# Three small groups of matmuls of a fused attention and feed-forward kernel, moved into one place of its hand-written order

## The chip, the cores and the metric

The kernel runs on one core of a Trainium2 chip. The metric is the device time of one execution in microseconds; lower is better. Times are given as the median of several runs.

## What is computed

From `reference.py`, cut to what matters. Shapes: q, k, v (8, 8, 576, 64), p (8, 8, 32, 64); all float32.

```python
def sm_attn(qq, kk, vv):
    s = scale * np.matmul(qq, kk.transpose(0, 1, 3, 2))
    s = s - np.max(s, axis=-1, keepdims=True)
    a = np.exp(s)
    a = a / (np.sum(a, axis=-1, keepdims=True) + 1e-09)
    return np.matmul(a, vv)
p_packed = sm_attn(p, k, v)            # 32 packed rows per head
out = sm_attn(q, p_packed, p_packed)   # 576 tokens per head
# out -> x of (4608, 512), then _moe_ref and _moe2_ref:
xn = x / sqrt(mean(x * x) + 1e-06) * rms_g
g = xn @ w_gate                        # 512 x 1536
val = xn @ w_val
x = (g * sigmoid(g) * val) @ w_out     # 1536 x 512
h = x @ w_in                           # 512 x 2048
return (maximum(h, 0) + alpha * minimum(h, 0)) @ w_out2
```

## The kernel before, in words

There are two stages. The first works through the 8 batches, each in two half tiles of 288 tokens (`tile(b, half, at)`); the second stage, a loop over 9 tiles of 512 tokens, isn't touched. The order of each engine's work is written out by hand, engine by engine, and the engines meet at semaphores.

A half tile is a loop over f, the 12 chunks of 128 hidden columns. For each f TensorE computes a gate product (6 large matmuls of 288 columns into PSUM bank 0) and a val product (6 more, bank 1). Each large product is three passes of a high and a low part (`three_passes`, lines 580 to 582). ScalarE takes the silu of the gate (line 964), VectorE multiplies it with val ("mult", line 1213), ScalarE rounds the result to its high part ("h_hi", line 970), VectorE subtracts for the low part ("h_lo", line 1216). From f=2 on TensorE follows with the down product of chunk f-2: 12 large matmuls into the four y banks, 4 to 7. The next gate waits for the silu before it, the next val for the mult before it, since each has only one bank. At the end of a half tile VectorE and ScalarE evict the y banks (lines 1224, 978, 980) and SyncE stores them.

The weights of the gate and val products are not w_gate and w_val. Since the second attention's probabilities times the packed rows come ahead of them, the kernel multiplies the weights by the packed rows first: the six weight products of a batch, `fold0` to `fold5`, each 8 small matmuls of 512 columns on 64x32 tiles of the array (line 712; a float32 matmul has two records in the trace, so 16). They go to banks 2 and 3 and are cast to `m_hi` (ScalarE, line 929) and subtracted to `m_lo` (VectorE, line 1163), two instructions on each engine. fold5 makes chunks 10 and 11.

While batch b is in its tiles, the attention of batch c = b + 1 is prepared between the large matmuls. Tables say at which place which step stands: `PE_PLACES`, `DVE_PLACES`, `ACT_PLACES`, keyed by (half, where, f), with "ready" (ahead of the last three val matmuls), "within" (behind the gate), "after" (behind the val product), "between" (behind the down product). `PE_FIRST` and its like add the late steps of batch 0 in the first tile. The steps that matter here:

- `scores0`, `scores1`: the two halves of p times k, each 8 small matmuls of 288 columns on 64x32 tiles (line 600), in banks 2 and 3 at f=1 and f=2 of half 0. ScalarE copies each half to `a_sb` (line 871).
- `max0`, `max1` at f=2: VectorE's maximum over `a_sb` and a small scaling (lines 1040, 1043). `exp0`, `exp1` behind f=3: ScalarE's exponentials (line 876), which need another activation table than silu, so there is a table load ahead of them and one ahead of silu 4.
- `split(b, 1)`: the high (ScalarE, line 917, at f=1) and low part (VectorE, line 1156, at f=2) of the second half's activations.
- `fold5` of batch c at (1, "between", 11), the end of half 1.

A run of steps on small tiles between large matmuls is called a visit below.

Of the kernel before, what the change touches and what calls it, by code (L numbers as in the profile page):

```python
# [15 lines left out]
PACK = 32  # L16
# [24 lines left out]
PE_PLACES = {  # L41
    (0, "ready", 1): ["scores0_ready"], (0, "after", 1): ["scores0"],
    (0, "ready", 2): ["scores1_ready"], (0, "after", 2): ["scores1"],
    (0, "after", 5): ["turn_a01"], (0, "between", 5): ["turn_a2"], (0, "between", 6): ["packed"],
# [9 lines left out]
}  # L54
# [9 lines left out]
    (1, "between", 8): ["fold3"], (1, "within", 10): ["split0"], (1, "between", 10): ["fold4"],  # L64
    (1, "between", 11): ["fold5"],
}
ACT_PLACES = {
    (0, "between", 1): ["scores0"], (0, "between", 2): ["scores1"], (0, "after", 3): ["exp0", "exp1"],
    (0, "between", 5): ["turn_a0"], (0, "within", 6): ["turn_a2"],
    (0, "within", 8): ["packed"], (0, "after", 11): ["probs"], (0, "between", 11): ["silu"],  # L70
    (1, "between", 1): ["fold0"], (1, "between", 3): ["fold1"], (1, "after", 6): ["rsqrt"], (1, "between", 6): ["fold2"],
    (1, "between", 8): ["fold3"], (1, "between", 9): ["split0"], (1, "between", 10): ["fold4"], (1, "between", 11): ["fold5"],
}
# [8 lines left out]
ACT_FIRST = {  # L82
    (0, "after", 0): ["fold5", "fold4"], (0, "between", 6): ["rsqrt1"], (0, "within", 9): ["split1"],
}
EARLY_BANK, LATE_BANK = 7, 0
# [9 lines left out]
def build(nc, q_t, k_t, v_s, p_t, w1_gv, w1_o, w2, rms_g, alpha, out_t):  # L95
# [3 lines left out]
    with ExitStack() as ctx:  # L99
# [137 lines left out]
        gate_ps, val_ps = psum[:, 0, 0:HALF], psum[:, 1, 0:HALF]  # L237
        scores_ps = psum[:, 2:4, 0:HALF]
        pp_ps, ppt_ps = psum[:, 3, 0:P], psum[:, 2, 0:P]
# [4 lines left out]
        def first(c):  # L244

            return isinstance(c, int) and c == 0
# [27 lines left out]
        def m_bank(c, j):  # L274

            return [4, 6, 4, 2, 6, 4][j] if first(c) else 2

        def scores0_of(g):
# [69 lines left out]
        def tiles_of_a(eng, tile, beside):  # L348

            table, starting = {"PE": (PE_PLACES, PE_FIRST), "DVE": (DVE_PLACES, DVE_FIRST),  # L350
                               "Activation": (ACT_PLACES, ACT_FIRST)}[eng.engine.name]

            def places_of(c, half):
                def at(where, f):
                    if c == 1:
                        for name in starting.get((half, where, f), []):
                            beside(0, name)
                    if c < BATCH:
                        for name in table.get((half, where, f), []):
                            beside(c, name)  # L360
                return at

            for b in range(BATCH):
                for half in range(2):
                    tile(b, half, places_of(b + 1, half))
# [211 lines left out]
        def _(pe):  # L577
# [6 lines left out]
            def scores_ready(c, h):  # L584

                pe.wait_ge(k_in[h], 16 * (c + 1))
                if h == 0:
                    pe.wait_ge(p_in, 16 * (c + 1))
                    if c > 0:
                        pe.wait_ge(m_lo_done, evicted(c))  # L590
                elif c > 0:
                    pe.wait_ge(scores_out, 2 * (c - 1) + 1)

            def scores(c, h):

                for pair in range(PAIRS):
                    for e in range(2):
                        dims = slice(HEAD_DIM * e, HEAD_DIM * (e + 1))
                        dst = psum[PACK * pair:PACK * (pair + 1), 2 * e + h if first(c) else 2 + e, 0:HALF]
                        mm = nc.tensor.matmul(dst, p_sb[dims, pair, :],  # L600
                                              k_sb[dims, pair, h * HALF:(h + 1) * HALF], start=True, stop=True)
                mm.then_inc(scores_mm, 1)

            def turn_a(c, t):

                if t == 0:
                    pe.wait_ge(a_normed, GROUPS * (c + 1))
                    reached(pe, mean_copied, 2 * c)
                if t == 2 and c > 0:
                    pe.wait_ge(at_act, 2 * c + 1)  # L610
# [105 lines left out]

            def beside(c, name):
                if name in ("scores0_ready", "scores1_ready"):
                    scores_ready(c, int(name[6]))
# [40 lines left out]
            def tile(b, half, at):  # L760
                n = 2 * b + half
                for f in range(NF1 + LAG):
# [26 lines left out]
                    if f >= LAG:  # L789
                        d = f - LAG  # L790
                        if n == 0 and d == 0:
                            pe.wait_ge(m_raw_done, len(RAW_M))
                        if d == 0:
                            pe.wait_ge(y_act, 2 * n + 2)
                            pe.wait_ge(y_dve, 2 * n + 2)
# [69 lines left out]
        def _(act):  # L865
            def scores_copy(c, h):

                act.wait_ge(scores_mm, 2 * c + h + 1)
                if h == 0 and c > 1:
                    act.wait_ge(a2n_done, 2 * c)  # L870
                nc.scalar.copy(a_sb[:, :, h * HALF:(h + 1) * HALF], scores_ps).then_inc(scores_out, 1)

# [58 lines left out]

            def beside(c, name):
                if name in ("scores0", "scores1"):
                    scores_copy(c, int(name[-1]))
# [360 lines left out]
```

## Time and profile before

| | |
|---|---|
| time, median of 3 runs | 1558.12 us (1558.12 to 1561.55) |
| the profiled execution's own time | 1559.83 us |
| its span in the profile | 1558.0 us |
| TensorE (PE) busy | 1545.6 us, 99% |
| VectorE (DVE) busy | 729.1 us, 47% |
| ScalarE (ACT) busy | 445.8 us, 29% |
| GpSimd (POOL) busy | 196.3 us, 13% |

Busy means that an instruction of the engine was running; matmuls are pipelined and their ends are modelled, so one instruction's time overlaps the next one's, and the distance between two starts says more than either duration. The span is the time between the first and the last record of the profiled execution.

### The profile page before, as it was taken

What the parts mean: (1) busy time and instruction counts of PE and PEld (TensorE: products, weight loads), DVE (VectorE), ACT (ScalarE), POOL (GpSimd) and SP (SyncE); (2) the same over time, 40 slices, a digit from 0 to 9 for tenths busy, and PEclk for the clock granted to TensorE, in tenths of its full rate; (3) what the DMA queues carried; (4) which work ended last, traced back from release to release, by engine and by line L of the source; (5) the groups of instructions that cost most, each with busy time, mean ns of one, the idle gap of its engine ahead of it and who ended that gap; (6) DMA issues with size and microseconds to landing.
All of it is one profiled execution on the core that took longest, in us unless ns stands there. A gap on an engine that the chain in (4) does not pass through costs nothing.

```text
span 1558.0 us, 25676 instructions
## 1 busy us (share of the span) xinstructions
PE 1545.6 (99%) x10324; PEld 1318.6 (85%) x10324; DVE 729.1 (47%) x1281; ACT 445.8 (29%) x847; POOL 196.3 (13%) x186
## 2 busy tenths in 40 slices
PE   8999999999999999999999999999999999999999
PEld 3888889889898989889988888888888888888887
DVE  5765554646556455554443333333343333333343
ACT  3545344443534445342211111111111111111111
POOL 2710000000000000007561002020201002020000
PEclk9999999999999999999999999999999999999999
DMA  9212102021210302003300001010100001010000
GB/s 352 89 38 79 47 27 84 16 79 47 79 47 1 105 21 77 17 17 151 139 13 28 27 0 54 0 54 0 44 10 27 27 9 45 0 54 0 27 0 27
DMA packets 42739, 76.16 MB, mean 49 GB/s; under 512 B 2209, under 2 KB 19617, under 8 KB 42657
## 3 DMA queue, kind: packets, MB, share of 16 engines
q1 hardware_dynamic: 37760, 66.08, 12.4%
q10 hardware_dynamic: 4896, 8.92, 1.5%
q8 instruction: 61, 1.00, 0.3%
q14 instruction: 22, 0.17, 0.0%
HBM read 56.11 MB, written 18.87 MB: 48 GB/s over the span
## 4 chain that ended last, share of the span: by engine, by line
PE 96%; DVE 3%; ACT 1%; issue 1%; POOL 0%; DVEq 0%; POOLq 0%; ACTq 0%
PE psum L580 30%; PE psum L581 29%; PE psum L582 29%; PE psum L712 3%; PE psum L674 1%; PE psum L806 1%; PE psum L614 1%; PE psum L600 1%; PE psum L629 1%; PE psum L662 0%; PE psum L681 0%; DVE act_sb L1213 0%; DVE h_lo L1216 0%; DVE e L1086 0%; DVE e L1071 0%
## 5 line engine op out<-in xcount | busy, mean ns | idle before, releaser
L1249 DVE TENSOR_TENSOR h_lo<-g,h_hi 128x512 fp32r<-128x512 f32 x144 | 107.3, 745 | 470.2 <-ACT h_hi L997 470.2
L997 ACT CAST h_hi<-g 128x512 fp32r<-128x512 f32 x144 | 89.4, 621 | 633.4 <-PE psum L582 599.0
L580 PE MATMUL psum<-an_hi,m_hi 128*128 128x288 f32 x768 | 236.8, 308 | 2.4 <-DVE an_lo L1156 1.0
L580 PE MATMUL psum<-h_hi,ow_hi 128*128 128x288 f32 x768 | 233.0, 303 | 0.6 <-DVE h_lo L1216 0.6
L581 PE MATMUL psum<-an_hi,m_lo 128*128 128x288 f32 x768 | 226.4, 295 | 0.0
L582 PE MATMUL psum<-an_lo,m_hi 128*128 128x288 f32 x768 | 226.3, 295 | 0.0
L582 PE MATMUL psum<-h_lo,ow_hi 128*128 128x288 f32 x768 | 225.8, 294 | 0.0
L581 PE MATMUL psum<-h_hi,ow_lo 128*128 128x288 f32 x768 | 225.7, 294 | 0.0
L580 PEld LDWEIGHTS psum<-h_hi,ow_hi 128*128 128x128 f32 x768 | 144.0, 188 | 35.0 <-issue 34.1
L580 PEld LDWEIGHTS psum<-an_hi,m_hi 128*128 128x128 f32 x768 | 144.6, 188 | 24.0 <-issue 17.3
L1213 DVE TENSOR_TENSOR act_sb<-act_sb,psum 128x288 f32<-128x288 f32 x192 | 86.0, 448 | 160.9 <-PE psum L582 143.1
L1216 DVE TENSOR_TENSOR h_lo<-act_sb,h_hi 128x288 fp32r<-128x288 f32 x192 | 106.0, 552 | 108.3 <-ACT h_hi L970 108.3
L581 PEld LDWEIGHTS psum<-an_hi,m_lo 128*128 128x128 f32 x768 | 144.8, 189 | 1.1
L582 PEld LDWEIGHTS psum<-an_lo,m_hi 128*128 128x128 f32 x768 | 144.7, 188 | 0.0
L581 PEld LDWEIGHTS psum<-h_hi,ow_lo 128*128 128x128 f32 x768 | 144.2, 188 | 0.1
L582 PEld LDWEIGHTS psum<-h_lo,ow_hi 128*128 128x128 f32 x768 | 144.1, 188 | 0.0
L580 PE MATMUL psum<-h_hi,w_hi_front 128*128 128x512 f32 x360 | 140.7, 391 | 0.0
L582 PE MATMUL psum<-h_lo,w_hi_front 128*128 128x512 f32 x360 | 140.1, 389 | 0.0
L581 PE MATMUL psum<-h_hi,w_lo_front 128*128 128x512 f32 x360 | 140.1, 389 | 0.0
L581 PE MATMUL psum<-xs,w_lo_front 128*128 (+1 forms) x360 | 140.1, 389 | 0.0
L580 PE MATMUL psum<-xs,w_hi_front 128*128 (+1 forms) x360 | 140.1, 389 | 0.0
L582 PE MATMUL psum<-xs,w_hi_front 128*128 (+1 forms) x360 | 140.0, 389 | 0.0
(141 smaller groups left out, 2390.9 us busy)
## 6 DMA issues: line engine op xcount, KB each, us to landing
k_sb<-k_t SPq DMA_DIRECT2D x16, 576.0 KB, 5.0
q_sb<-q_t SPq DMA_DIRECT2D x8, 1152.0 KB, 5.9
y_mid<-y_sb SPq DMA_DIRECT2D x16, 576.0 KB, 3.5
xs_raw<-y_mid SPq DMA_DIRECT2D x9, 1024.0 KB, 5.1
out_t<-o_sb ACTq DMA_DIRECT2D x34, 256.0 KB, 2.0
v_sb<-v_s SPq DMA_DIRECT2D x8, 1024.0 KB, 6.6
gv_sb<-w_gv SPq DMA_DIRECT2D x4, 1536.0 KB, 18.7
w_raw_front<-w SPq DMA_DIRECT2D x2, 2560.0 KB, 12.6
```

The costliest lines, as they stand in the source:

```text
L580: nc.tensor.matmul(dst, w_hi, hi, start=start, stop=False)
L581: nc.tensor.matmul(dst, w_lo, hi, start=False, stop=False)
L582: return nc.tensor.matmul(dst, w_hi, lo, start=False, stop=stop)
L600: mm = nc.tensor.matmul(dst, p_sb[dims, pair, :], k_sb[dims, pair, h * HALF:(h + 1) * HALF], start=True, stop=True)
L614: mm = nc.tensor.transpose(at_ps(c, t)[:, at:at + P], a_sb[:, g, KEY_STARTS[j]:KEY_STARTS[j] + P], ident[:])
L629: mm = nc.tensor.matmul(pp_ps[PACK * pair:PACK * (pair + 1), e * HEAD_DIM:(e + 1) * HEAD_DIM], a_t[:, j, col:col + PACK], v_sb[:, j, head ...
L674: mm = nc.tensor.matmul(psum[:, gram_bank(c, h) + e, 0:HALF], gram_sb[:, e, :], a2[:, h, e, :], start=True, stop=True)
L712: mm = nc.tensor.matmul(psum[keys, m_bank(c, j) + e, :].rearrange("p (f n) -> p f n", f=2), pp_tg[dims, pair, :], gv_sb[dims, 2 * j:2 * j ...
L997: nc.scalar.copy(h2_hi[:, f % 2, :], g32[:, f % 2, :]).then_inc(g_hi_done, 1)
L1213: nc.vector.tensor_tensor(act_sb[:, s, :], act_sb[:, s, :], val_ps, ALU.mult).then_inc(h32_done, 1)
L1216: nc.vector.tensor_tensor(h_lo[:, s, :], act_sb[:, s, :], h_hi[:, s, :].bitcast(F32), ALU.subtract).then_inc(h_lo_done, 1)
L1249: nc.vector.tensor_tensor(h2_lo[:, s, :], g32[:, s, :], h2_hi[:, s, :].bitcast(F32), ALU.subtract).then_inc(g_lo_done, 1)
```

## The change

fold5 of batches 1 to 7 leaves the end of half 1 and goes behind the gate and val products of f=0 in the first half tile of its own batch (table `CARRIED`). For batches 2 to 7 both halves of the scores leave f=1 and f=2 and follow it at the same place, as one step `scores`. They go to the y banks (4, 5 and 6, 7), so they wait until the half tile before has been evicted, and the first down product waits until both are copied out. ScalarE copies both halves at f=0 and casts fold5 at f=1; VectorE subtracts for fold5 at f=1. Batch 1 keeps its scores where they were (table `SECOND`). The rows of `an_hi`, `an_lo`, `h_hi` and `h_lo` are 1280 bytes apart (288 + 32 floats) in both kernels; the diff does not touch them.

```diff
--- before.py
+++ after.py
@@ -39,8 +39,7 @@
 SUM_EPS, RMS_EPS = 1e-9, 1e-6
 
 PE_PLACES = {
-    (0, "ready", 1): ["scores0_ready"], (0, "after", 1): ["scores0"],
-    (0, "ready", 2): ["scores1_ready"], (0, "after", 2): ["scores1"],
+    (0, "after", 0): ["scores"],
     (0, "after", 5): ["turn_a01"], (0, "between", 5): ["turn_a2"], (0, "between", 6): ["packed"],
     (0, "after", 7): ["turn_packed"],
     (0, "ready", 8): ["tokens0_ready"], (0, "after", 8): ["tokens0"],
@@ -50,7 +49,6 @@
     (1, "between", 5): ["means"], (1, "ready_down", 6): ["fold2_ready"], (1, "between", 6): ["fold2"],
     (1, "ready", 8): ["fold3_ready"], (1, "after", 8): ["fold3"],
     (1, "ready", 10): ["fold4_ready"], (1, "after", 10): ["fold4"],
-    (1, "ready_down", 11): ["fold5_ready"], (1, "between", 11): ["fold5"],
 }
 DVE_PLACES = {
     (0, "between", 2): ["max0", "max1"], (0, "between", 3): ["norm0"],
@@ -62,14 +60,13 @@
     (1, "after", 4): ["turn_p1"], (1, "between", 4): ["weigh1"],
     (1, "within", 6): ["means"], (1, "between", 6): ["fold2"], (1, "between", 7): ["newton"],
     (1, "between", 8): ["fold3"], (1, "within", 10): ["split0"], (1, "between", 10): ["fold4"],
-    (1, "between", 11): ["fold5"],
 }
 ACT_PLACES = {
-    (0, "between", 1): ["scores0"], (0, "between", 2): ["scores1"], (0, "after", 3): ["exp0", "exp1"],
+    (0, "between", 0): ["scores"], (0, "after", 3): ["exp0", "exp1"],
     (0, "between", 5): ["turn_a0"], (0, "within", 6): ["turn_a2"],
     (0, "within", 8): ["packed"], (0, "after", 11): ["probs"], (0, "between", 11): ["silu"],
     (1, "between", 1): ["fold0"], (1, "between", 3): ["fold1"], (1, "after", 6): ["rsqrt"], (1, "between", 6): ["fold2"],
-    (1, "between", 8): ["fold3"], (1, "between", 9): ["split0"], (1, "between", 10): ["fold4"], (1, "between", 11): ["fold5"],
+    (1, "between", 8): ["fold3"], (1, "between", 9): ["split0"], (1, "between", 10): ["fold4"],
 }
 PE_FIRST = {
     (0, "ready", 0): ["fold5_ready"], (0, "after", 0): ["fold5", "fold4_ready", "fold4"], (0, "after", 3): ["gram1"], (0, "after", 4): ["mean1"],
@@ -81,6 +78,17 @@
 }
 ACT_FIRST = {
     (0, "after", 0): ["fold5", "fold4"], (0, "between", 6): ["rsqrt1"], (0, "within", 9): ["split1"],
+}
+SECOND = {
+    "PE": {(0, "ready", 1): ["scores0_ready"], (0, "after", 1): ["scores0"],
+           (0, "ready", 2): ["scores1_ready"], (0, "after", 2): ["scores1"]},
+    "DVE": {},
+    "Activation": {(0, "between", 1): ["scores0"], (0, "between", 2): ["scores1"]},
+}
+CARRIED = {
+    "PE": {(0, "ready", 0): ["fold5_ready"], (0, "after", 0): ["fold5"]},
+    "DVE": {(0, "between", 1): ["fold5"]},
+    "Activation": {(0, "between", 1): ["fold5"]},
 }
 EARLY_BANK, LATE_BANK = 7, 0
 FILLERS = {"scores0": (3, EARLY_BANK), "scores1": (1, EARLY_BANK), "turn_a01": (4, EARLY_BANK),
@@ -235,7 +243,6 @@
 
         psum = ctx.enter_context(nc.psum_tensor("psum", [P, 8, BANK], F32))
         gate_ps, val_ps = psum[:, 0, 0:HALF], psum[:, 1, 0:HALF]
-        scores_ps = psum[:, 2:4, 0:HALF]
         pp_ps, ppt_ps = psum[:, 3, 0:P], psum[:, 2, 0:P]
 
         def s2_ps(e):
@@ -274,6 +281,10 @@
         def m_bank(c, j):
 
             return [4, 6, 4, 2, 6, 4][j] if first(c) else 2
+
+        def scores_bank(c, h, e):
+
+            return [2 * e + h, 2 + e, 4 + 2 * h + e][min(c, 2)]
 
         def scores0_of(g):
 
@@ -352,11 +363,17 @@
 
             def places_of(c, half):
                 def at(where, f):
+                    place = (half, where, f)
                     if c == 1:
-                        for name in starting.get((half, where, f), []):
+                        for name in starting.get(place, []):
                             beside(0, name)
+                        for name in SECOND[eng.engine.name].get(place, []):
+                            beside(1, name)
+                    else:
+                        for name in CARRIED[eng.engine.name].get(place, []):
+                            beside(c - 1, name)
                     if c < BATCH:
-                        for name in table.get((half, where, f), []):
+                        for name in table.get(place, []):
                             beside(c, name)
                 return at
 
@@ -586,17 +603,20 @@
                 pe.wait_ge(k_in[h], 16 * (c + 1))
                 if h == 0:
                     pe.wait_ge(p_in, 16 * (c + 1))
-                    if c > 0:
-                        pe.wait_ge(m_lo_done, evicted(c))
-                elif c > 0:
-                    pe.wait_ge(scores_out, 2 * (c - 1) + 1)
+                if c == 1 and h == 0:
+                    pe.wait_ge(m_lo_done, evicted(1))
+                elif c == 1:
+                    pe.wait_ge(scores_out, 1)
+                elif c > 1 and h == 0:
+                    pe.wait_ge(y_act, 4 * (c - 1) + 2)
+                    pe.wait_ge(y_dve, 4 * (c - 1) + 2)
 
             def scores(c, h):
 
                 for pair in range(PAIRS):
                     for e in range(2):
                         dims = slice(HEAD_DIM * e, HEAD_DIM * (e + 1))
-                        dst = psum[PACK * pair:PACK * (pair + 1), 2 * e + h if first(c) else 2 + e, 0:HALF]
+                        dst = psum[PACK * pair:PACK * (pair + 1), scores_bank(c, h, e), 0:HALF]
                         mm = nc.tensor.matmul(dst, p_sb[dims, pair, :],
                                               k_sb[dims, pair, h * HALF:(h + 1) * HALF], start=True, stop=True)
                 mm.then_inc(scores_mm, 1)
@@ -606,6 +626,7 @@
                 if t == 0:
                     pe.wait_ge(a_normed, GROUPS * (c + 1))
                     reached(pe, mean_copied, 2 * c)
+                    reached(pe, m_lo_done, evicted(c))
                 if t == 2 and c > 0:
                     pe.wait_ge(at_act, 2 * c + 1)
                 for j in range(2 * t, min(2 * t + 2, CHUNKS)):
@@ -715,6 +736,10 @@
                 mm.then_inc(m_mm, 1)
 
             def beside(c, name):
+                if name == "scores" and c > 1:
+                    for h in range(2):
+                        scores_ready(c, h)
+                        scores(c, h)
                 if name in ("scores0_ready", "scores1_ready"):
                     scores_ready(c, int(name[6]))
                 if name in ("scores0", "scores1"):
@@ -790,6 +815,8 @@
                         d = f - LAG
                         if n == 0 and d == 0:
                             pe.wait_ge(m_raw_done, len(RAW_M))
+                        if d == 0 and half == 0 and 1 < b + 1 < BATCH:
+                            pe.wait_ge(scores_out, 2 * (b + 1))
                         if d == 0:
                             pe.wait_ge(y_act, 2 * n + 2)
                             pe.wait_ge(y_dve, 2 * n + 2)
@@ -868,7 +895,8 @@
                 act.wait_ge(scores_mm, 2 * c + h + 1)
                 if h == 0 and c > 1:
                     act.wait_ge(a2n_done, 2 * c)
-                nc.scalar.copy(a_sb[:, :, h * HALF:(h + 1) * HALF], scores_ps).then_inc(scores_out, 1)
+                bank = scores_bank(c, h, 0)
+                nc.scalar.copy(a_sb[:, :, h * HALF:(h + 1) * HALF], psum[:, bank:bank + 2, 0:HALF]).then_inc(scores_out, 1)
 
             def scores_exp(c, g):
 
@@ -930,6 +958,9 @@
                                    psum[:, m_bank(c, j) + e, :].rearrange("p (f n) -> p f n", f=2)).then_inc(m_hi_done, 1)
 
             def beside(c, name):
+                if name == "scores" and c > 1:
+                    scores_copy(c, 0)
+                    scores_copy(c, 1)
                 if name in ("scores0", "scores1"):
                     scores_copy(c, int(name[-1]))
                 if name in ("exp0", "exp1"):
```

## Rows read from the trace of the kernel before

**Rows 1.** The page: busy time of each engine, and the chain by engine.

```profile
PE 1545.6 (99%) x10324; PEld 1318.6 (85%) x10324; DVE 729.1 (47%) x1281; ACT 445.8 (29%) x847; POOL 196.3 (13%) x186
...
PE 96%; DVE 3%; ACT 1%; issue 1%; POOL 0%; DVEq 0%; POOLq 0%; ACTq 0%
```

**Rows 2.** Windows: length, busy time of each engine, clock, DMA.

```profile
231.30:324.30 93.00, 92.95 (x857) 82.92 (x857) 50.95 (x107) 42.21 (x85) 3.55 (x3) 1.00 0.16 53
```

**Rows 3.** Timeline of TensorE around fold5: start, length in us.

```profile
223.89 0.29 PE L582 MATMUL psum<-h_lo,ow_hi 128*128 128x288 f32 x1
224.12 1.09 PE L712 MATMUL psum<-gv_sb,pp_tg 64*32 64x512 f32 x16
225.14 0.40 PE L580 MATMUL psum<-h_hi,ow_hi 128*128 128x288 f32 x1
225.37 0.29 PE L581 MATMUL psum<-h_hi,ow_lo 128*128 128x288 f32 x1
```

**Rows 4.** Timeline of TensorE in the first half tile.

```profile
37.82 1.95 PE L712 MATMUL psum<-gv_sb,pp_tg 64*32 64x512 f32 x32
39.70 0.40 PE L580 MATMUL psum<-an_hi,m_hi 128*128 128x288 f32 x1
...
41.26 0.29 PE L582 MATMUL psum<-an_lo,m_hi 128*128 128x288 f32 x1
41.48 0.72 PE L600 MATMUL psum<-k_sb,p_sb 64*32 64x288 f32 x16
42.12 0.40 PE L580 MATMUL psum<-an_hi,m_hi 128*128 128x288 f32 x1
42.36 0.30 PE L581 MATMUL psum<-an_hi,m_lo 128*128 128x288 f32 x1
```

**Rows 5.** Timeline of TensorE, half 0 of batch 2.

```profile
228.40 0.30 PE L580 MATMUL psum<-an_hi,m_hi 128*128 128x288 f32 x1
...
231.53 0.29 PE L582 MATMUL psum<-an_lo,m_hi 128*128 128x288 f32 x1
...
237.16 0.29 PE L582 MATMUL psum<-an_lo,m_hi 128*128 128x288 f32 x1
...
242.69 0.29 PE L582 MATMUL psum<-h_lo,ow_hi 128*128 128x288 f32 x1
243.03 0.37 PE L580 MATMUL psum<-an_hi,m_hi 128*128 128x288 f32 x1
243.24 0.29 PE L581 MATMUL psum<-an_hi,m_lo 128*128 128x288 f32 x1
```

**Rows 6.** Timeline of ScalarE, from the end of batch 1 on.

```profile
225.31 1.07 ACT L929 CAST m_hi<-psum 128x512 fp32r<-128x512 f32 x2 [1.68 <-PE psum L712]
...
228.60 0.40 ACT L980 COPY y_sb<-psum 128x288 f32<-128x288 f32 x1
...
232.42 0.43 ACT L970 CAST h_hi<-act_sb 128x288 fp32r<-128x288 f32 x1 [0.94 <-DVE act_sb L1213]
232.75 0.63 ACT L871 COPY a_sb<-psum 128x576 f32<-128x576 f32 x1
233.28 0.68 ACT L917 CAST an_hi<-a 128x576 fp32r<-128x576 f32 x1
233.86 0.41 ACT L964 ACTIVATE act_sb<-psum 128x288 f32<-128x288 f32 x1
...
237.49 0.41 ACT L964 ACTIVATE act_sb<-psum 128x288 f32<-128x288 f32 x1 [1.68 <-PE psum L582]
...
242.47 0.41 ACT L964 ACTIVATE act_sb<-psum 128x288 f32<-128x288 f32 x1
```

**Rows 7.** Timeline of VectorE over the same stretch.

```profile
225.93 1.29 DVE L1163 TENSOR_TENSOR m_lo<-psum,m_hi 128x512 fp32r<-128x512 f32 x2 [1.80 <-ACT m_hi L929]
...
234.35 0.45 DVE L1213 TENSOR_TENSOR act_sb<-act_sb,psum 128x288 f32<-128x288 f32 x1 [1.01 <-ACT act_sb L964]
...
238.35 0.45 DVE L1213 TENSOR_TENSOR act_sb<-act_sb,psum 128x288 f32<-128x288 f32 x1
```

## The prediction

> **What bounds the kernel now.** I read the page first. TensorE is busy for 99% of the span and carries 96% of the chain that ended last [rows 1]. The windows of one period of the first stage (93.0 us, two tiles) show TensorE busy for 92.95 us at a granted clock of 1.00; six such windows, one after another from 138.3 us on, read the same 92.95 (the second of them stands in [rows 2]). So the time is the sum of what TensorE issues, plus short holds that "busy" hides, because the modelled end of a matmul overlaps the next. I therefore read the starts in the timeline and not the busy times. In a dense stretch two starts of 288 columns are 0.13 us apart. What matters is each place where they are not.
>
> Such places are of two kinds. One is a visit to the 64x32 tiles. Around the old sixth weight product (fold5) the last large matmul starts at 223.89 and the second large one behind the visit at 225.37, 1.48 us where two steps take 0.26: the visit costs 1.22 us [rows 3]. A half of the scores costs 42.36 - 41.26 - 0.26 = 0.84 us [rows 4]. The other kind is a hold on data. At the end of f=4 in half 0, gate 5 starts 0.34 us behind the last down matmul and its follower 0.21 us later, instead of 0.13 each: 0.29 us lost; ahead of it 42 dense steps, from 237.16 to 242.69, are 0.1317 each [rows 5]. It waits for silu 4, which ScalarE does only after a table load, two exponentials and another table load: 4.98 us from silu 3 to silu 4 [rows 6].
>
> **The change, part by part.** Twelve visits go. For batches 2 to 7 each batch had three (fold5 of the batch before, scores 0, scores 1) and gets one: 2 x 6 = 12. Batch 1 keeps its two score visits, batch 0's fold5 stays, and fold5 of batch 7 keeps a visit of its own, only at another place.
>
> The price of a joined group. Two weight products in one visit lie in the trace (the start of the first tile): first small matmul at 37.82, first large one at 39.70, 1.88 us, where one alone takes 225.14 - 224.12 = 1.02. The second adds 0.86 [rows 3, 4]. The wait instructions between those two cost nothing visible, since both their semaphores had long been reached. For the scores no joined row exists. A score group alone takes 42.12 - 41.48 = 0.64 us for 288 columns, a fold 1.02 for 512: 0.0017 us per column and 0.15 fixed. So 288 columns joined add 0.49, or by scaling 0.86 with the columns, 0.48. I take 0.48; the bounds are 0.48 and 0.64 (nothing shared). The joined visit then costs 1.22 + 2 x 0.48 = 2.18 us against 1.22 + 2 x 0.84 = 2.90: 0.72 us saved per batch, 4.3 us over six.
>
> One rule speaks against this. The Trainium skill, "TensorE: Matmul & The Clock Gate", section "The mechanism" of the part on packing, says that weight loads overlap running matmuls only when their row group is another one; a group joined behind another uses the same row groups, so its loads would be exposed. By the page's figure of columns / 1.2 ns, an estimate of 27 ns for each of two passes of two joined groups, six visits would give back 0.6 us. The trace does not agree: by the 0.0017 us per column above, 512 columns are 0.87 us, and the second fold adds 0.86, so nothing but columns.
>
> The waits move too. In the joined visit TensorE meets, between fold5 and the scores, waits for the key and p loads and for all four y banks evicted (the scores now land in the y banks). With zero at the tile's start, 228.40, fold5 starts at about 1.67 and the scores at 2.55; ScalarE's last y copy starts at 0.20 (228.60) and takes 0.40 [rows 5, 6]. Nearly 2 us to spare: price nothing; without that cover each 0.1 us late is 0.6 us in all. The key load was issued after the tokens product of the half tile before last, tens of us earlier. The new wait at down 0 (both score copies done) is reached at 7.0, the copies end near 5.0: nothing. The queue of SyncE gets its turn for q and the next p some 3 us earlier than now; their users come at f=8 and in the next batch: nothing.
>
> What ScalarE and VectorE now do. Before: a score copy behind h_hi 1 and one behind h_hi 2. After: both copies behind h_hi 0, and the two fold5 casts (VectorE: two subtractions) behind h_hi 1, ahead of the split cast and silu 2. Behind silu 2 VectorE has mult 2, h_lo 2, two maxima with their scalings, the other split and only then mult 3. I follow this chain in a tile of half 0 with the rows' distances:
> - The second gate-1 matmul starts at 1.45 (last of f=0, 11 steps) + 2.18 + 0.26 = 3.89, the last of val 1 at 5.20. Silu 1 finds ScalarE free: the score copies start near 3.3 and 3.8, end by 4.5 in pitch, and silu 1 is wanted at 4.74 (last gate matmul 4.41, and 237.49 - 237.16 = 0.33 for the release).
> - h_hi 1 follows the last val matmul by 232.42 - 231.53 = 0.89: 6.09. The next instruction follows in 0.33: 6.42. The two casts take 1.08 us less 0.1 overlap: 7.40. The split cast takes 0.58 (233.28 to 233.86): silu 2 at 7.98, where its gate was ready at 6.4 [rows 5, 6].
> - From silu 2 to mult 3 the trace has 0.49 + 4.00 = 4.49 us (233.86, 234.35, 238.35), and all of it is VectorE's own string of work [rows 6, 7]. So mult 3 starts at 12.47 and ends at 12.92. The two fold5 subtractions (1.29 us for both, the first begun behind the first cast) are done just before mult 2 and push nothing.
> - TensorE: f=2 has the small loss that f=1 has now (23 steps from 228.40 are 3.02, the trace has 3.13: 0.11; the visit now lies behind f=0 and no longer behind f=1, so this loss moves and stays). Last val 2 at 6.88, down 0 to 8.46, gate 3 at 8.59. Silu 2 ends at 8.39, which with 0.15 of release is 8.54: just in time. Val 3 to 10.04, down 1 to 11.62, gate 4 to 12.41, and val 4 wants to start at 12.54. It overwrites the bank mult 3 reads, so it starts at 12.92 + 0.10 to 0.15, and its follower loses 0.07 more: a hold of 0.45 to 0.6 us, I take 0.55. Now this hold does not exist: a score visit and its copy lie between silu 2 and this place, and mult 3 (238.35) has more than 1 us to spare.
> - Given back: silu 3 at 9.59, silu 4 at 14.57 to 14.7, ready at 15.1; gate 5 now wants 15.46. The old hold of 0.29 us at gate 5 is gone.
>
> Net of holds 0.55 - 0.29 = 0.26 us in six tiles: 1.6 us. In batch 7's half tile there are no maxima and no exponential, so the fold5 visit is only moved: nothing. At the end of half 1 the fold5 visit leaves; down 11 then comes 1.2 us sooner, but h_lo 11 is ready about 1 us ahead of it still, and ScalarE and VectorE lose the fold5 work there. The second stage does not change; its weights are split more than 15 us ahead of use.
>
> **Sum.** 4.3 - 1.6 = 2.7 us less. The profiled execution took 1559.83 us for a span of 1558.0; its like should take 1557.1 with a span of 1555.3. The median of the three runs is 1558.12, at the span and not at 1559.83, so the median forecast is 1555.4 us (ratio 0.9983). A change under 0.3% (4.7 us) is about what a measurement of this kernel cannot tell from none.
>
> **Rivals.**
> (a) TensorE stays dense: val 4's hold is no more than the 0.29 us that it replaces at gate 5, since the gate-5 hold gives it back. For it: the hold is the small difference of two long chains, and 0.26 us less on ScalarE does it. Against it: every duration in the chain repeats over the batches. Then the whole 4.3 us stays: 1553.8.
> (b) The joined score groups share nothing but the mode switch, 0.64 each instead of 0.48, because the inline waits keep the weights from being loaded ahead: 0.32 x 6 = 1.9 us back, and 1557.3. Against it stands the joined fold pair with waits in it.
> (c) Slower: ScalarE's fold5 casts hold silu 2 far enough that val 4 is held for more than 0.29 + 0.72 = 1.01 us; from there on the change loses, and from 1.8 us on it loses over 0.3%. For it: the score copies, casts and split now stand in one strict order on ScalarE, and one instruction that waits for an unseen semaphore holds all. If the casts came behind one more half gate (0.8 us later) the hold would be 1.35 us, the loss 2.0 us: 1560.2. Against it: their inputs are ready 3 us before.
> (d) The change does what it says but the visits' cost was only hiding data holds, so that all 4.3 us reappear as holds: 1558.1. For it is the value of one such hold worked out above; against it that no other place comes out short.
>
> **How the numbers follow.** Forecast (holds of 0.3 to 0.8, gain 1.3 to 4.2) 0.56; (a) 0.20; (b) 0.09; (c) 0.06; (d) 0.09. From 1553.0 (case a with 0.5 to 1 us of holds that vanish elsewhere) to 1558.2 (case d) holds about 8 in 10; the forecast's own range is 1554.0 to 1556.8. Over 0.3% faster needs 0.4 us more than case (a) gives: 0.10. Over 0.3% slower is the far half of (c) and a shift of the runs: 0.04. Within: 0.86.
>
> **What would show it.** In the changed profile: one visit behind f=0 of half 0 in batches 1 to 6, with 48 small matmuls, about 2.0 us from first small to first large start, (b) if it is 2.2 or more. Behind it, silu 2 at about 7.98 from the tile's start, directly behind the split cast. At 12.5 to 13.1 a gap of 0.5 to 0.65 us between gate 4's last and val 4's first matmul start (0.13 in case a, over 1.1 in case c), and no gap at gate 5. The period falls from 93.0 to 92.55 us. The forecast is wrong if another hold opens, most likely at gate 3, which I find 0.05 us on the safe side.

## The result, and the profile after

The changed kernel takes 1554.66 us (median of 11 runs, 1554.32 to 1556.79); the kernel before took 1558.12 in the same comparison (11 runs, 1557.66 to 1561.55). The ratio is 0.9977, with a 95% interval of 0.9968 to 0.9987: a gain of 3.5 us, near the 2.7 us forecast and inside the range. It is under the 0.3% that the prediction took for the limit of what can be told from none, yet the interval lies below 1, so with 11 runs of each kernel it can be told. The profiled execution took 1554.32 us for a span of 1552.5; the one of before took 1559.83 for 1558.0. These two differ by 5.5 us, 2 us more than the medians, and the first thing to settle is which microseconds belong to the change.

The page of the changed kernel answers to [rows 1]: TensorE still sets the end, and it is busy 6.0 us less for the same 10324 matmuls.

```profile
PE 1539.6 (99%) x10324; PEld 1318.5 (85%) x10324; DVE 728.0 (47%) x1281; ACT 446.4 (29%) x847; POOL 196.0 (13%) x186
...
PE 96%; DVE 3%; ACT 1%; issue 1%; POOL 0%; DVEq 0%; POOLq 0%; ACTq 0%
```

The window of one period (length, busy time of each engine, clock, DMA) answers to [rows 2]: over a window of 92.30 us in place of 93.00 TensorE is again busy throughout, at a clock of 1.00.

```profile
226.90:319.20 92.30, 92.30 (x863) 83.18 (x855) 50.77 (x106) 42.33 (x85) 3.56 (x3) 1.00 0.17 53
```

TensorE's timeline at the joined visit, then at f=4 of the same half tile (batch 2, whose first large matmul starts at 224.35), answers to [rows 3 to 5].

```profile
224.35 0.30 PE L597 MATMUL psum<-an_hi,m_hi 128*128 128x288 f32 x1
...
225.80 0.29 PE L599 MATMUL psum<-an_lo,m_hi 128*128 128x288 f32 x1
226.03 1.09 PE L733 MATMUL psum<-gv_sb,pp_tg 64*32 64x512 f32 x16
226.91 1.18 PE L620 MATMUL psum<-k_sb,p_sb 64*32 64x288 f32 x32
228.01 0.40 PE L597 MATMUL psum<-an_hi,m_hi 128*128 128x288 f32 x1
228.25 0.30 PE L598 MATMUL psum<-an_hi,m_lo 128*128 128x288 f32 x1
...
236.78 0.30 PE L599 MATMUL psum<-an_lo,m_hi 128*128 128x288 f32 x1
236.97 0.40 PE L597 MATMUL psum<-an_hi,m_hi 128*128 128x288 f32 x1
237.21 0.30 PE L598 MATMUL psum<-an_hi,m_lo 128*128 128x288 f32 x1
...
239.33 0.29 PE L599 MATMUL psum<-h_lo,ow_hi 128*128 128x288 f32 x1
239.50 0.37 PE L597 MATMUL psum<-an_hi,m_hi 128*128 128x288 f32 x1
239.71 0.29 PE L598 MATMUL psum<-an_hi,m_lo 128*128 128x288 f32 x1
```

The visit: 228.25 - 225.80 less two steps of 0.13 is 2.19 us for fold5 and both halves of the scores, where three visits took 2.90. From the first small to the first large matmul are 1.98 us. Then the two holds: at val 4 (236.97) the starts are 0.19 and 0.24 apart (0.17 us lost over two steps of 0.13), at gate 5 (239.50) 0.17 and 0.21 (0.12 us lost). Together they are 0.29 us, just what gate 5 alone lost before [rows 5].

ScalarE and VectorE in the same half tile (timeline), to be read against [rows 6, 7]:

```profile
227.71 1.18 ACT L899 COPY a_sb<-psum 128x576 f32<-128x576 f32 x2 [0.59 <-PE psum L620]
...
230.46 0.43 ACT L1001 CAST h_hi<-act_sb 128x288 fp32r<-128x288 f32 x1 [0.93 <-DVE act_sb L1244]
230.79 1.07 ACT L957 CAST m_hi<-psum 128x512 fp32r<-128x512 f32 x2
231.75 0.68 ACT L945 CAST an_hi<-a 128x576 fp32r<-128x576 f32 x1
232.32 0.42 ACT L995 ACTIVATE act_sb<-psum 128x288 f32<-128x288 f32 x1
```

```profile
232.78 0.45 DVE L1244 TENSOR_TENSOR act_sb<-act_sb,psum 128x288 f32<-128x288 f32 x1
233.73 0.46 DVE L1247 TENSOR_TENSOR h_lo<-act_sb,h_hi 128x288 fp32r<-128x288 f32 x1 [0.50 <-ACT h_hi L1001]
234.11 0.75 DVE L1071 TENSOR_REDUCE negmax<-a_sb 128x1 f32<-128x576 f32 x1
...
234.96 0.75 DVE L1071 TENSOR_REDUCE negmax<-a_sb 128x1 f32<-128x576 f32 x1
...
235.81 0.75 DVE L1187 TENSOR_TENSOR an_lo<-a,an_hi 128x576 fp32r<-128x576 f32 x1
236.47 0.45 DVE L1244 TENSOR_TENSOR act_sb<-act_sb,psum 128x288 f32<-128x288 f32 x1
```

Silu 2 starts at 232.32, 7.97 us into the tile (forecast 7.98), straight behind the split cast. Mult 3 starts at 12.12 (forecast 12.47).

**Where the 5.5 us went.** I compared the starts of the same large matmul in both timelines. The difference, changed minus before, is:

| place | before | changed | difference |
|---|---|---|---|
| last val matmul of f=0, half 1 of batch 0 | 88.37 | 86.25 | -2.12 |
| last val matmul of f=11, half 0 of batch 1 | 174.91 | 172.08 | -2.83 |
| same, batch 6 | 640.00 | 633.66 | -6.34 |
| same, batch 7 | 726.72 | 720.30 | -6.43 |
| first matmul of the second stage | 770.29 | 764.82 | -5.47 |
| last matmul | 1554.32 | 1548.81 | -5.51 |

Three parts stand out. The first 2.1 us arise before any changed instruction. The windows of the first tile (before, then changed; the clock is the third figure from the right) show it:

```profile
35.00:40.00 5.00, 5.00 (x46) 3.33 (x46) 2.43 (x5) 1.98 (x5) 4.84 (x6) 0.72 1.05 382
```

```profile
35.00:40.00 5.00, 5.00 (x67) 2.82 (x66) 2.43 (x6) 2.62 (x5) 4.84 (x6) 1.00 1.04 382
```

TensorE ran these 5 us at a mean granted clock of 0.72 in the one execution and 1.00 in the other, so it left its low level (1.2 GHz) earlier. That isn't the change: the runs of each kernel, too, lie in two groups about 2 us apart (the changed one eight times at 1554.3 to 1555.3 and three times at 1556.5 to 1556.8), and the profile of before happened to be of the upper group. The ten profiles of this document bear the link with the clock out: three are of an upper group (before, scores joined, all together), and from 36 to 38 us these three show a clock of 0.50 to 0.54, the other seven 1.00. Then come 0.71 us in each of six batches, 4.2 in all. And in the last half tile of the first stage the change loses 0.96 us, which I had not foreseen. With 0.1 us more in batch 7, 4.2 + 0.1 - 1.0 = 3.3 us is about what the medians show (3.5).

The loss in the last half tile, first TensorE, then VectorE, then GpSimd (timelines of the changed kernel):

```profile
729.08 0.30 PE L599 MATMUL psum<-an_lo,m_hi 128*128 128x288 f32 x1
730.74 0.40 PE L597 MATMUL psum<-an_hi,m_hi 128*128 128x288 f32 x1 [1.36 <-DVE act_sb L1244]
```

```profile
727.98 2.35 DVE L1247 TENSOR_TENSOR h_lo<-act_sb,h_hi 128x288 fp32r<-128x288 f32 x1 [0.50 <-ACT h_hi L1001]
730.25 0.44 DVE L1244 TENSOR_TENSOR act_sb<-act_sb,psum 128x288 f32<-128x288 f32 x1
```

```profile
727.62 2.38 POOL L572 TENSOR_TENSOR w_lo_front<-w_raw_front,w_hi_front 128x1024 fp32r<-128x1024 f32 x1
```

VectorE's h_lo 0, a subtraction of two operands in SBUF that takes 0.46 us elsewhere, takes 2.35 us and ends 0.3 us after a GpSimd subtraction of the second stage's weight split. Mult 1 stands behind it and ends at 730.69. The matmul at 729.08 is the last of gate 2, and val 2 waits for mult 1, since it overwrites the bank that mult 1 reads: it starts 1.66 us behind gate 2 instead of 0.13. In the kernel before, the same pair overlaps less, and val 2 starts 0.70 us behind gate 2:

```profile
734.40 1.40 DVE L1216 TENSOR_TENSOR h_lo<-act_sb,h_hi 128x288 fp32r<-128x288 f32 x1 [0.50 <-ACT h_hi L970]
```

```profile
733.08 2.40 POOL L555 TENSOR_TENSOR w_lo_front<-w_raw_front,w_hi_front 128x1024 fp32r<-128x1024 f32 x1
```

### The profile page after: what moved, and what is told of

Same layout as the page of the kernel before. It is cut to its first block, busy times and chain, and to the rows that moved or that the text cites. A ratio compares the mean times of both kernels' runs of the same rounds, so it can differ in the third digit from the quotient of the medians.

```text
span 1552.5 us, 25676 instructions
## 1 busy us (share of the span) xinstructions
PE 1539.6 (99%) x10324; PEld 1318.5 (85%) x10324; DVE 728.0 (47%) x1281; ACT 446.4 (29%) x847; POOL 196.0 (13%) x186
## 4 chain that ended last, share of the span: by engine, by line
PE 96%; DVE 3%; ACT 1%; issue 1%; POOL 0%; DVEq 0%; POOLq 0%; ACTq 0%
PE psum L597 30%; PE psum L598 29%; PE psum L599 29%; PE psum L733 3%; PE psum L695 1%; PE psum L635 1%; PE psum L650 1%; PE psum L833 1%; PE psum L683 0%; PE psum L620 0%; PE psum L702 0%; DVE act_sb L1244 0%; DVE h_lo L1247 0%; DVE e L1117 0%; DVE e L1102 0%
```

## The experiments

The ratio is to the kernel before. Totals hold two things that are not the question, the start (two groups 2 us apart) and the overlap in the last half tile, so the main reading is the period of a batch, from the starts of the same matmul (last val of f=11, half 0) in five consecutive batches. Within one trace these periods agree within 0.03 us. The last column is the distance from the last val matmul of f=1 to that of f=2 in the last half tile of the first stage; without a hold it is 1.67.

| kernel | median us | ratio to before, 95% | period us | f=1 to f=2, last half tile |
|---|---|---|---|---|
| before | 1558.12 | | 93.02 | 2.26 |
| changed | 1554.66 | 0.9977 [0.9968, 0.9987] | 92.31 | 3.22 |
| scores joined, fold5 at its old place | 1555.98 | 0.9987 [0.9978, 0.9996] | 92.66 | 2.36 |
| two visits at f=0 | 1557.09 | 0.9995 [0.9986, 1.0004] | 92.67 | 3.26 |
| three visits at f=0 | 1561.46 | 1.0024 [1.0015, 1.0033] | 93.30 | 3.26 |
| split late | 1554.59 | 0.9979 [0.9970, 0.9988] | 92.30 | 3.36 |
| GpSimd waits | 1553.53 | 0.9971 [0.9959, 0.9983] | 92.32 | 1.67 |
| before, GpSimd waits | 1557.64 | 0.9997 [0.9988, 1.0006] | 93.01 | 1.68 |
| longer VectorE string | 1558.91 | 1.0007 [0.9998, 1.0016] | 92.99 | 3.38 |
| all together | 1553.18 | 0.9961 [0.9948, 0.9975] | 92.00 | 1.69 |

**Scores joined, fold5 at its old place.** The tables of before get fold5 back (TensorE's line is the first, VectorE's and ScalarE's are alike), and `CARRIED` is empty.

```diff
+    (1, "ready_down", 11): ["fold5_ready"], (1, "between", 11): ["fold5"],
...
+    (1, "between", 11): ["fold5"],
...
-    "PE": {(0, "ready", 0): ["fold5_ready"], (0, "after", 0): ["fold5"]},
-    "DVE": {(0, "between", 1): ["fold5"]},
-    "Activation": {(0, "between", 1): ["fold5"]},
+CARRIED = {"PE": {}, "DVE": {}, "Activation": {}}
```

> Only the two halves of the scores are joined at f=0; fold5 stays at the end of half 1 as in the kernel before. Theory V (a visit to the small tiles has a price of its own of about 0.36 us, wherever it stands): the period of one batch (93.02 us before, 92.31 in the changed kernel) is 92.66, one visit short of each; over six batches 2.1 us less than before. With the two fold5 casts away from f=1, silu 2 comes 0.96 us earlier, so val 4 isn't held and gate 5 is held for 0.29 us again, which changes the period by nothing. Rival O (the gain comes from the new order on ScalarE and VectorE, not from TensorE's visits): the period stays near 93.0 or falls to 92.3 with the score copies moved, not to the middle.

Measured: the period is 92.66, as theory V has it, and half the gain. In its trace val 4 isn't held, and the starts at gate 5 are 0.34 and 0.21 us apart as before.

**Two visits and three visits at f=0.** TensorE's order alone is changed, back towards separate visits, without moving them away: the first pair of lines makes two visits, and the second pair makes three of them (cut: two lines that let `half0` and `half1` name one half of `scores` each).

```diff
-    "PE": {(0, "ready", 0): ["fold5_ready"], (0, "after", 0): ["fold5"]},
+    "PE": {(0, "within", 0): ["fold5_ready", "fold5"]},
...
-    (0, "after", 0): ["scores"],
+    (0, "ready", 0): ["half0"], (0, "after", 0): ["half1"],
```

> The changed kernel with fold5 behind the gate product of f=0 and the scores behind the val product: TensorE's joined visit is cut in two with six large matmuls between, the other engines keep their order. Theory V: the period is 92.31 + 0.36 = 92.67 us and the six batches take 2.2 us more than in the changed kernel. Rival O: the period stays at 92.31.

> As the run with two visits, and the first half of the scores ahead of the last three val matmuls of f=0, so three visits with large matmuls between, the other engines' order unchanged. Theory V: the period is 92.31 + 0.72 = 93.03, that of the kernel before, and the whole gain is gone. Rival O: it stays at 92.31. Rival P (a visit costs only when a weight load of a large matmul is late behind it, so that three large matmuls between two visits would hide part): between 92.67 and 93.03.

Measured: two visits have a period of 92.67, 0.35 us more, as V has it; O falls. The timeline of TensorE shows the second entry and exit:

```profile
318.75 1.09 PE L733 MATMUL psum<-gv_sb,pp_tg 64*32 64x512 f32 x16
...
320.00 0.30 PE L598 MATMUL psum<-an_hi,m_lo 128*128 128x288 f32 x1
...
320.53 0.29 PE L599 MATMUL psum<-an_lo,m_hi 128*128 128x288 f32 x1
320.75 1.20 PE L620 MATMUL psum<-k_sb,p_sb 64*32 64x288 f32 x32
321.88 0.40 PE L597 MATMUL psum<-an_hi,m_hi 128*128 128x288 f32 x1
```

Three visits have 93.30, 0.27 more than V's 93.03, and by its median the kernel is slower than the one before (ratio 1.0024). The extra has a place of its own. Only one visit is now left between the end of val 0 and gate 1, so mult 0, h_hi 0 and both score copies end late, and silu 1 starts at 231.44 straight behind them (in the changed kernel it finds ScalarE idle). Gate 2 waits for it: the starts are 0.44 and 0.21 apart, 0.39 us lost, where the changed kernel loses 0.10 at f=2. The visits themselves can be read one by one. Here are the second and the third (TensorE's timeline, with the small matmuls of each cut):

```profile
227.91 0.29 PE L599 MATMUL psum<-an_lo,m_hi 128*128 128x288 f32 x1
...
229.01 0.30 PE L598 MATMUL psum<-an_hi,m_lo 128*128 128x288 f32 x1
229.15 0.29 PE L599 MATMUL psum<-an_lo,m_hi 128*128 128x288 f32 x1
...
230.26 0.29 PE L598 MATMUL psum<-an_hi,m_lo 128*128 128x288 f32 x1
```

Less two steps of 0.13 they cost 0.84 and 0.85 us, as much as a half of the scores alone [rows 4], though only three large matmuls lie between them; the first costs 1.22. That is 2.91 us for three visits, against 2.55 for two and 2.19 for one: 0.36 each, and the three large matmuls hide nothing. P falls.

**Split late.** ScalarE's place first, then VectorE's.

```diff
-                    if half == 0 and f == 1 and b > 0:
+                    if half == 0 and f == (6 if b < BATCH - 1 else 1) and b > 0:
                         split(b, 1)
...
-                    if half == 0 and f == 2 and b > 0:
+                    if half == 0 and f == (7 if b < BATCH - 1 else 2) and b > 0:
                         split(b, 1)
```

> The changed kernel with the split of the second half's activations (0.58 us of ScalarE at f=1, about 0.7 us of VectorE at f=2) at f=6 and f=7, in batches 1 to 6. Theory G (the hold at val 4, 0.17 us, was only carved out of the hold at gate 5, 0.12 us, which the exponentials set): val 4 isn't held, gate 5 is held for 0.29 us, the period stays at 92.31 within 0.03. Rival H (the two holds add up, each from its own cause): the period falls by 0.17 to 92.14, 1.0 us over six batches.

Measured: 92.30, no gain. The hold at val 4 is gone and the whole 0.29 us is back at gate 5 (TensorE's timeline, 0.34 us between these starts):

```profile
331.48 0.29 PE L599 MATMUL psum<-h_lo,ow_hi 128*128 128x288 f32 x1
331.83 0.37 PE L597 MATMUL psum<-an_hi,m_hi 128*128 128x288 f32 x1
```

G holds: what is taken from the one is given back at the other. H falls.

**GpSimd waits**, in the changed kernel and in the one before.

```diff
                 nc.gpsimd.tensor_copy(hi, whole).then_inc(w2_hi_done, 1)
                 pool.wait_ge(w2_hi_done, f + 1)
+                if f == 6:
+                    pool.wait_ge(h_lo_done, NF1 * (2 * BATCH - 1) + 2)
                 nc.gpsimd.tensor_tensor(lo, whole, hi.bitcast(F32), ALU.subtract).then_inc(w2_ready, 1)
```

> The changed kernel with one wait on GpSimd: the seventh subtraction of its weight split for the second stage starts only when VectorE's h_lo 1 of the last half tile is done. In the changed kernel that subtraction runs from 727.62 to 730.01 and h_lo 0 of the last half tile, which starts at 727.98, takes 2.35 us instead of 0.46; gate 2 then starts 1.66 us behind val 1 instead of 0.13. Theory L (VectorE's subtraction from SBUF is locked out while GpSimd's runs): h_lo 0 takes 0.46 us, the gap is gone and the kernel is 1.5 us faster than the changed one. Rival S (something else delays the start of the last half tile, the two only coincide): the gap stays near 1.6 us and the time too.

> The kernel before with the same wait on GpSimd. There the two subtractions overlap less: h_lo 0 takes 1.40 us and the gap is 0.70 us. Theory L: the gap goes and the kernel gets 0.55 us faster than the kernel before; so the difference between the changed kernel and the one before, each without the overlap, is 4.3 us plus what the start differs. Rival S: the same time as before.

The gap that the expectation puts between val 1 and gate 2 is the one between gate 2 and val 2 shown above.

Measured: with GpSimd held back, h_lo 0 of the last half tile takes 0.46 us (VectorE, then GpSimd, changed kernel with the wait):

```profile
728.79 0.46 DVE L1249 TENSOR_TENSOR h_lo<-act_sb,h_hi 128x288 fp32r<-128x288 f32 x1 [0.50 <-ACT h_hi L1003]
```

```profile
731.07 2.41 POOL L574 TENSOR_TENSOR w_lo_front<-w_raw_front,w_hi_front 128x1024 fp32r<-128x1024 f32 x1 [2.53 <-DVE h_lo L1249]
```

The step from f=1 to f=2 falls from 3.22 to 1.67 us in the changed kernel and from 2.26 to 1.68 in the one before. The medians fall by 1.1 and 0.5 us. L holds for the mechanism and S falls; of the 1.5 us forecast for the changed kernel 0.4 are missing. In the profile with the wait the same thing happens to h_lo 11 of the half tile before (2.07 us from 722.11, where the changed kernel's profile has 1.53), and the last down product waits for it (0.41 and 0.21 between starts, 0.36 us lost). Without this overlap the two kernels differ by 1557.64 - 1553.53 = 4.1 us.

**Longer VectorE string.** The split's subtraction is done twice.

```diff
+                    if half == 0 and f == 2 and 0 < b < BATCH - 1:
+                        dve.wait_ge(an_hi_done, 2 * b + 2)
+                        nc.vector.tensor_tensor(an_lo[:, 1], a2[:, 1], an_hi[:, 1].bitcast(F32), ALU.subtract).then_inc(twice, 1)
+                        dve.wait_ge(twice, b)
                     if half == 0 and f == 2 and b > 0:
                         split(b, 1)
```

> The changed kernel with VectorE's split of the second half's activations done twice in batches 1 to 6 (about 0.75 us more ahead of mult 3); the result is the same. Theory G (mult 3 sets val 4's start, and the wait there first takes up the 0.29 us that gate 5 would be held for): val 4's hold grows from 0.17 to about 0.9, gate 5's goes from 0.12 to 0, the period rises by 0.6 us to 92.9 and six batches cost 3.8 us: this is the loss that I had forecast, in another size. Rival N (VectorE is off the path there): the period stays at 92.31.

Measured: the period is 92.99, 0.68 more (forecast 0.6), for an instruction that adds 0.78 us (two starts of the subtraction, 329.61 and 330.39). TensorE's timeline:

```profile
330.59 0.29 PE L600 MATMUL psum<-an_lo,m_hi 128*128 128x288 f32 x1
331.57 0.40 PE L598 MATMUL psum<-an_hi,m_hi 128*128 128x288 f32 x1 [0.69 <-DVE act_sb L1245]
331.81 0.30 PE L599 MATMUL psum<-an_hi,m_lo 128*128 128x288 f32 x1
...
333.93 0.29 PE L600 MATMUL psum<-h_lo,ow_hi 128*128 128x288 f32 x1
334.06 0.29 PE L598 MATMUL psum<-an_hi,m_hi 128*128 128x288 f32 x1
```

Val 4 loses 0.85 + 0.11 = 0.96 us, gate 5 nothing (0.13): 0.96 against 0.29 is 0.67, the whole rise. N falls. A loss of the kind that I had forecast exists, at the place named, once the string is long enough, and takes up gate 5's hold first.

**All together.** The late splits, the wait on GpSimd, and, in half 0 of batches 1 to 6 (`swap`), silu 4 ahead of h_hi 3 on ScalarE and h_lo 3 behind mult 4 on VectorE:

```diff
+                    if swap and f == 3:
+                        silu(4)
...
                     at("after", f)
+                    if swap and f == 4:
+                        low(3)
+                    if not (swap and f == 3):
+                        low(f)
```

> A version meant to beat both: the changed kernel with the late splits, the wait on GpSimd, and in half 0 of batches 1 to 6 silu 4 ahead of h_hi 3 on ScalarE and mult 4 and the second normalization ahead of h_lo 3 on VectorE. Theory G: silu 4 comes 0.43 us sooner, which is more than the 0.29 us that gate 5 is held for, so no hold is left at val 4 and gate 5: the period falls to 92.03, 1.7 us over six batches, and with the 1.5 us of the last half tile the kernel is 3.2 us faster than the changed one, 1551.4. Rival R (another hold opens behind, at the turn of the scores behind f=5 or at down 3, since h_lo 3 is later by 2 us): the period stays at 92.3 or rises.

Measured: the period is 92.00 and TensorE has no hold at val 4 or gate 5. Silu 4 stands ahead of h_hi 3 (ScalarE; the first line is silu 3):

```profile
327.94 0.41 ACT L997 ACTIVATE act_sb<-psum 128x288 f32<-128x288 f32 x1 [0.41 <-PE psum L601]
...
332.61 0.41 ACT L997 ACTIVATE act_sb<-psum 128x288 f32<-128x288 f32 x1
332.92 0.42 ACT L1011 CAST h_hi<-act_sb 128x288 fp32r<-128x288 f32 x1
```

Silu 4 starts 4.67 us behind silu 3 instead of 4.98. That is 0.31 us sooner and not the 0.43 forecast, just enough for the 0.29 us that gate 5 was held. R falls.

The median is 1553.18, ratio 0.9961 [0.9948, 0.9975]; the runs lie at 1551.0 to 1551.5 (two) and 1553.2 to 1553.5 (three), the two groups of the start. Group for group it is 3.3 us below the changed kernel (1551.0 against 1554.3), near the 3.2 forecast. By medians it is 1.5 us below, and the two intervals overlap (the changed kernel's is 0.9968 to 0.9987). Against the kernel before, the whole interval is below 1.

## Why the prediction was right, point by point

- **The visits.** Forecast 2.18 us for the joined visit against 2.90; measured 2.19. The runs with two and three visits, in which nothing moves but TensorE's order, put 0.35 to 0.36 us on each visit. So this is the cause of the 0.71 us per batch, not only a sum that agrees with it. The Trainium skill, "TensorEngine Tiling (Array Packing)", section "Key Properties", says that a change of the tiling mode drains the engine. The trace fits it, with 0.36 us for one entry and exit together, but no run tells a drain from another cost of going in and out.
- **The joined score groups** were taken at 0.48 us each from a scaled row: right (the joined visit takes 1.98 us from first small to first large start, fold5 alone 1.02, so 0.48 for each half); rival (b) at 0.64 is out. The rule on weight loads of the same row group, from the Trainium skill, "TensorE: Matmul & The Clock Gate", section "The mechanism", would have made the joined visit 0.1 us longer by the estimate in the prediction. The trace does not agree: 0.48 us for 288 columns and 0.86 for 512 are both 0.0017 us per column, with nothing left for a load.
- **The waits that moved cost nothing.** Behind the joined visit, up to gate 5, no start is late but those forecast at f=2 (0.10 us in all) and gate 3 (0.01), and the two named; the first down product follows val 2 at once.
- **Silu 2** comes at 7.97, as worked out (7.98): the chain over the score copies, casts and split cast holds to 0.01 us. Gate 3, called just in time, lost 0.01.
- **The term that was mis-sized is the hold at val 4**: 0.55 forecast, 0.17 measured. The step that fails is that all of the 4.49 us from silu 2 to mult 3 "is VectorE's own string of work". The string did not run without pauses in the kernel before. Its timeline, ScalarE's second score copy first, then VectorE:

```profile
235.17 0.64 ACT L871 COPY a_sb<-psum 128x576 f32<-128x576 f32 x1
```

```profile
235.30 0.46 DVE L1216 TENSOR_TENSOR h_lo<-act_sb,h_hi 128x288 fp32r<-128x288 f32 x1 [0.50 <-ACT h_hi L970]
235.84 0.75 DVE L1040 TENSOR_REDUCE negmax<-a_sb 128x1 f32<-128x576 f32 x1
...
237.55 0.75 DVE L1156 TENSOR_TENSOR an_lo<-a,an_hi 128x576 fp32r<-128x576 f32 x1
```

The first maximum started 0.54 us behind the start of h_lo 2, since it waited for the second score copy to end (235.81); now both copies are long done and the distance is 0.38 (233.73 to 234.11). And mult 3 (238.35) started 0.80 us behind the split's subtraction because it waited for val 3: it stood 0.41 us behind val 3's last matmul (237.94), as mult 1 stood 0.40 behind val 1's. Now the distance is 0.66 (235.81 to 236.47). These two waits are 0.30 of the 0.34 us by which 4.49 became 4.15. The rest of the miss is the release, 0.05 us from the end of mult 3 (236.92) to val 4 (236.97) and not 0.10 to 0.15.
- **The hold given back at gate 5** was right in kind: 0.29 became 0.12, and 0.17 + 0.12 is 0.29, so the move cost nothing. The net of 0.26 us per batch, 1.6 us in all, that the forecast took off was not there. Which of the two places holds does not matter until val 4 alone asks for more than 0.29 (the longer string). That is case (a), to which I gave 0.20: its 4.3 us are what the batches show (4.2).
- **What brought the total back to the forecast** is a loss on no list of mine, the overlap of h_lo 0 with GpSimd's subtraction in the last half tile, 0.96 us more than before. Forecast 2.7, made of 4.3 - 1.6; measured 3.5, made of 4.3 - 1.0 and what the medians scatter. That the median landed 0.7 us from the forecast is in part luck: two errors of opposite sign.
- Rivals (c) and (d) are out: no hold near 1.0 us in any batch, and the gain stays with the batches.

## What to carry to other kernels

A stay on another tile shape has a price for going in and out, here 0.36 us, that neither the number of matmuls in it nor three large matmuls between two of them change: put groups of the same shape side by side, and count the visits before anything else. When you move work, follow each engine's string to the next place where the bound engine waits, and ask of every distance that you take over from the old trace whether it is work or itself a wait: a wait for something that the change makes earlier goes away. Two holds on one chain need not add up: here the later one gave back what the earlier one took, as long as the earlier one was the shorter (0.17 against 0.29), and no more than its own 0.29 when it was longer (0.96).

## What the runs showed of the hardware that I had not expected

VectorE's subtraction of two SBUF operands (h_lo, 128x288 float32) takes 0.42 to 0.46 us alone. When a GpSimd subtraction of 128x1024 (2.4 to 2.7 us) is running as it starts, it ends 0.31 to 0.35 us behind that one, whatever is left of it: five to eight h_lo of batch 7 do so in each of the ten profiles, and the stretched ones take up to 2.71 us. GpSimd's cast between two subtractions does the same (an h_lo started at 712.17 in the changed kernel takes 1.02 us and ends 0.31 behind the cast). Mult, which reads one operand from PSUM, keeps its 0.44 to 0.46 in the same stretch. Moving GpSimd's instruction away brings 0.46 back. The Trainium skill, "SBUF — State Buffer", section "Who interferes with whom", states this: a VectorE instruction with two SBUF inputs contends with a GpSimd instruction that reads SBUF, because its second input comes through a read interface that the two share. The trace agrees, with 2.35 us against 0.46.

What the overlap costs depends on the phase. In the changed kernel h_lo 0 of the last half tile starts 0.36 us behind GpSimd's subtraction, in the kernel before 1.32 us behind it, and the shift of 0.96 us turned 0.6 us of lost TensorE time into 1.55. The other stretched h_lo of the same two profiles, of up to 2.60 us (at 718.60 in the kernel before), hold TensorE nowhere. The likely reason is that no down product lies behind f=0 and f=1 to cover the wait, as it does from f=2 on; no run tests that by itself.

The first tile's clock differs from one execution to the next: TensorE left its low level at 37.8 us in the profile of the kernel before and at 32.3 in that of the changed one, with 2.1 us between the two by f=0 of half 1 and the same instructions up to there. Earlier low stretches seem to cost nothing: the profile of the split late shows none at all from 25 to 40 us, and its last val matmul of f=0 in half 1 of batch 0 starts at 86.34, against 86.25 in the changed kernel, whose clock is 0.50 from 30 to 32 us. Why the low level comes when it does was not tested.
